# Token biases made behind the first row maxima, and two attention loads moved ahead of a larger one

## The reference

```python
def _attn_ref(q, k, v):                      # (2, 8, 768, 64) each
    k_sum = k.reshape(B, H, nb, 32, D).max(axis=3)
    v_sum = v.reshape(B, H, nb, 32, D).mean(axis=3)
    ...
    scores_all = np.concatenate([scores_l_m, scores_s], axis=-1)
    ...
    return np.matmul(a, np.concatenate([v, v_sum], axis=2))

def _moe_ref(x, modality_id, w_gate, modality_bias, w1, w2):
    logits = x @ w_gate + modality_bias[modality_id]
    e_idx = np.argmax(logits, axis=1)
    ...
            h = np.maximum(x[mask] @ w1[e], 0.0)
            out[mask] = gate_w[mask, None] * (h @ w2[e])

def _moe2_ref(x, w_in, w_out):
    h = np.maximum(x @ w_in, 0.0)
    return (h * h @ w_out).astype(np.float32)
```

## Time and profile before

| | us |
|---|---|
| three executions | 580.98, 581.5, 585.26 |
| median of them | 581.5 |
| the profiled execution, whole | 584.93 |
| its span | 583.3 |
| mean granted clock of PE in it | 0.959 |

### The profile page before, as it was taken

The page is one execution under the profiler, slowest core; times in us unless marked ns, Lnnn a source line. Parts: engine busy times, 40 slices in busy tenths (PEclk is TensorE's granted clock), DMA queues, the critical chain, the costliest instruction groups (busy, mean ns, idle before and its releaser), DMA issues.

```text
span 583.3 us, 9324 instructions
## 1 busy us (share of the span) xinstructions
PE 528.6 (91%) x3118; PEld 420.8 (72%) x3119; DVE 231.2 (40%) x434; ACT 187.5 (32%) x353; POOL 82.5 (14%) x100
## 2 busy tenths in 40 slices
PE   7878989959999699998369999999999999999996
PEld 3557778748888578786257888877888877888884
DVE  3785675966222242711552132233223224122222
ACT  1645764216221352711522222133122223122221
POOL 4423334200400040310450000011000000000000
PEclk9889988979999979999669999999999999999999
DMA  8987872691551017152220000004000001000001
GB/s 302 270 227 259 259 241 110 224 351 39 183 179 54 36 33 309 47 234 97 77 85 1 0 1 1 1 6 138 0 0 0 0 0 72 0 0 0 0 0 72
DMA packets 19272, 56.97 MB, mean 98 GB/s; under 512 B 2352, under 2 KB 2608, under 8 KB 18480
## 3 DMA queue, kind: packets, MB, share of 16 engines
q1 hardware_dynamic: 11888, 29.57, 15.9%
q0 software_dynamic: 4768, 23.60, 11.1%
q10 hardware_dynamic: 2592, 3.49, 1.6%
HBM read 42.49 MB, written 14.16 MB: 97 GB/s over the span
## 4 chain that ended last, share of the span: by engine, by line
PE 73%; issue 3%; DVE 3%; DMA 3%; ACT 3%; ACTq 1%; POOL 1%; DVEq 0%; POOLq 0%; SPq 0%
PE psum L1497 8%; PE psum L1498 8%; PE psum L1499 8%; PE psum L1478 7%; PE psum L1479 7%; PE psum L1480 7%; PE psum L1405 4%; PE psum L1406 4%; PE psum L1407 4%; PE psum L1388 4%; PE psum L1389 4%; PE psum L1390 4%; DMA x_in<-xs_d 2%; PE psum L1415 1%; ACT W L539 1%
## 5 line engine op out<-in xcount | busy, mean ns | idle before, releaser
L1187 DVE TENSOR_TENSOR sq<-r_sb 128x512 f32<-128x512 f32 x48 | 33.2, 693 | 156.7 <-ACT r_sb L650 156.7
L650 ACT ACTIVATE r_sb<-psum 128x512 f32<-128x512 f32 x48 | 28.8, 601 | 163.1 <-PE psum L1480 163.1
L1478 PE MATMUL psum<-z_hi,W 128*128 128x512 f32 x192 | 77.1, 401 | 0.8 <-DVE z_lo L1171 0.8
L1497 PE MATMUL psum<-W,s_hi 128*128 128x512 f32 x192 | 76.2, 397 | 1.1 <-DVE s_lo L1189 1.1
L1480 PE MATMUL psum<-z_hi,W 128*128 128x512 f32 x192 | 76.7, 399 | 0.0
L1479 PE MATMUL psum<-z_lo,W 128*128 128x512 f32 x192 | 76.7, 399 | 0.0
L1498 PE MATMUL psum<-W,s_hi 128*128 128x512 f32 x192 | 75.9, 396 | 0.0
L1499 PE MATMUL psum<-W,s_lo 128*128 128x512 f32 x192 | 75.8, 395 | 0.0
L1388 PE MATMUL psum<-W,x_hi 128*128 (+1 forms) x104 | 44.1, 425 | 7.6 <-DVE W L919 5.8
L1189 DVE TENSOR_TENSOR s_lo<-sq,s_hi 128x512 fp32r<-128x512 f32 x48 | 33.3, 693 | 33.6 <-ACT s_hi L652 33.6
L1405 PE MATMUL psum<-W,h_hi 128*128 (+1 forms) x104 | 42.9, 412 | 2.0 <-DVE h_lo L927 2.0
(11 more groups left out here) (198 smaller groups left out, 715.4 us busy)
## 6 DMA issues: line engine op xcount, KB each, us to landing
raw<-in_w POOLq DMA_DIRECT2D x4, 2048.0 KB, 12.3
raw<-in_w_io POOLq DMA_DIRECT2D x4, 2048.0 KB, 10.2
v_in<-in_v SPq DMA_DIRECT2D x12, 390.0 KB, 9.9
raw<-in_w SPq DMA_DIRECT2D x8, 512.0 KB, 10.2
kT<-in_kT SPq DMA_DIRECT2D x8, 400.0 KB, 7.4
q_in<-in_q SPq DMA_DIRECT2D x12, 256.0 KB, 7.9
X<-in_vT SPq DMA_DIRECT2D x2, 1536.0 KB, 14.5
x_in<-xs_d SPq DMA_DIRECT2D x12, 256.0 KB, 2.8
```

Source lines behind the costliest of these rows:

```text
L1478: pe.matmul(bank[f % 2][:, :], wh, z_hi[:, k, :], start=(k == 0), stop=False)
L1497: pe.matmul(bank[2 + j][:, :], s_hi[f % 2][:, tok], wh, start=(f == 0), stop=False)
```

## The change

In DVE's program, `bias_of_tokens()` moves from block 2 of the loop to the place behind `row_max(0)`, ahead of the loop. In SP's program, `load_v(3)` moves ahead of the second batch's vT, and `load_q(6)`, which stood behind `load_v(4)`, moves there too; in the loop that follows, the q asked for behind `load_v(i)` is that of block i + 3 instead of i + 2.

```diff
             load_q(5)
             load_v(2)
+            load_v(3)
+            load_q(6)
             load_values(1)
-            load_v(3)
             for i in range(VRING, NB):
                 load_v(i)
-                if i + 2 < NB:
-                    load_q(i + 2)
+                if i + RING < NB:
+                    load_q(i + RING)
                 if i == NBS:
                     sp.wait_ge(sem["zero"], 1)
...
             row_max(0)
+            bias_of_tokens()
             for i in range(NB):
                 if i + 1 < NB:
                     row_max(i + 1)
...
-                if i == 2:
-                    bias_of_tokens()
                 if i >= 2:
                     norm(i - 2)
```

## The result

The change makes the kernel a little faster: the median goes from 581.57 to 578.65 us (seven executions each), a ratio of 0.9935 with an interval of 0.9911 to 0.9958. The time lies in the range and within 1%, but the gain is some ten times the one forecast, and the interval of the ratio does not reach 1. The profiled execution after takes 580.0 us, the slowest of the seven; its span is 578.3, at a mean granted clock of 0.956.

The account below looks back on a forecast made before the run. PE's chain was taken to bound the kernel, with attention held up by the bias and the q_in load. A 1.3 us gain, limited by vT, and 1.0 us lost to the clock made -0.3: 581.2 us, range 578.5 to 585.2.

Parts of the forecast that it names:

- what follows attention only slides along: Stages after attention, ending near 88 us: the change touches none of them, so they only start earlier or later.
- What is late next: vT itself: Second batch's value sums: DVE waits 3.4 us for vT until 42.9, so gate(2) gains 1.3 us, not 3.87.
- the 40.5: vT's landing before the change, 23.30 + 17.2, taken from the profiled execution as the base for its new landing.
- the 2.4 us for 646 KB: DMA queue: v(3) and q(6) in front of vT delay its landing 2.4 us at 269 KB/us; bounds 0 and 2.7.
- the signs of being wrong: vT before 40.5, sum_values(1,0) without a wait, attention ending over 3 us earlier or 2 later, or changed dense stages.
- the 1.72 us for q_in: PE's wait at 44.45 for block 6's q load, expected to go because q(6) would land near 36.
- DVE's arrival: DVE reaches sum_values(1,0) at 39.45, moved by 2.15 us from 41.60, then waits for vT.
- The clock's +1.0 us: PE behind the vT wait: a hole of some 2.5 us lowers the clock and costs 1.0 us; bounds 0 and 1.7.
- The third: Rival at PE's vT wait: 1.2 GHz for twice as long costs 2.8 us; sum +1.5, 583.0 us; chance 0.18.
- the fourth: Rival: mbias late or bias still slow, row_max(1) up to 2.2 us late; 581.2 to 581.5 us; chance 0.04.
- the first (-1.3): Rival: PE's clock stays at 2.4 GHz behind the vT wait; -1.3 us, 580.2 us; chance 0.22.
- the second (-3.87): Rival: vT is not the new wait and both PE holes close; -3.87 us, 577.6 us; chance 0.08.

Follow-up runs that it names:

- the three profiles of the kernel after: The kernel with the whole change, measured three times without further edit, against the kernel before: ratios 0.9935, 0.9976 and 0.9948.
- again: The kernel before, profiled a second time with no edit: 581.24 us, span 579.6.
- all together: Kernel after with vT ahead of q(6) and v(3), sum_values(1,3) in block 5, four expert weight loads held back: 579.46 us, ratio 0.9933 against the kernel before.
- last sum: Kernel after with sum_values(1,3) moved from block 6 to block 5 on DVE: 578.78 us, ratio 0.9935 against the kernel before.
- twice: Kernel after with the six bias instructions made twice behind row_max(0): one profiled execution, 580.03 us.
- held: Kernel after with the first expert's last four weight loads held until the first token rows' scatters landed: 580.77 us, ratio 0.996 against the kernel before.

## Why the prediction was off

**Right, by the profile.** The bias costs 1.46 us at its new place (1.4 worked out), norm(0) comes at 27.20 (27.4), row_max(4) at 30.57 (30.77), mbias is there in time, and the hole in front of x_turn(0) closes. The wait for q_in goes. VT becomes what DVE waits for: 1.54, 0 and 2.76 us in the three profiles of the kernel after, where 3.4 was worked out. That what follows attention only slides along held to within the spread of single executions: from x_transpose(0) to the end it is 496.1 to 499.8 us in the fourteen profiles, before and after alike.

**The step that failed is "What is late next: vT itself"**, in its landing at 42.9. It has two terms, the 40.5 at which vT lands without the change and the 2.4 us for 646 KB put in front of it. It landed at 39.30, and two of the signs of being wrong that the forecast had named came: vT before 40.5, and an attention stage that ends over 3 us earlier. The trace records the landing of each of a transfer's 16 parts; the first, the fifteenth and the last of them for vT, in every profile:

```
moved in front of vT          first part        fifteenth         last part
nothing, v(3), v(4) next      32.10 31.84 31.33 35.85 35.05 35.97 40.52 38.00 39.09
  (before, again, bias alone)
nothing, q(6) next            31.82 31.54       35.64 34.20       35.68 35.01
  (vT first, all together)
q(6), 256 KB (v(3) behind)    33.25             37.27             37.35
v(3) and q(6), 646 KB         33.76 33.32 33.87 36.57 37.10 37.72 39.30 37.23 40.27
  (after x3, loads alone,     34.90 34.37 34.63 38.19 38.25 38.56 40.63 41.55 38.77
  last sum, twice, held)      33.93             37.95             38.65
v(3), q(6), v(4), 1036 KB     36.93             40.08             43.39
  (vT later, issued at 26.99)
```

The 2.4 us for the bytes hold for fifteen of the parts: from before's order to 646 KB in front, the mean of the first goes from 31.8 to 34.1 and that of the fifteenth from 35.6 to 37.8. What failed is the 40.5. DVE waits for the last part, and this one can stand alone behind the others: by 4.67 us in the profile of before, the widest of all, and by 2.73, 0.13 and 2.55 us in the three of the kernel after. The sum took the lag of one execution as the kernel's own; from the second profile of before, 38.00, it would have made 40.4. (The mean of the last part, 39.2 in three profiles and 39.5 in seven, does not tell 0.3 from 2.4, as single ones spread over 4 us.) The same error sits in the 1.72 us for q_in, 0.19 in the second profile of before. The forecast's own warning, that executions near 581 and near 585 exist, was applied to the total alone and not to the two landings.

The lag shows already in a load that stands in the queue ahead of those that the change moves. In the eight profiles in which the last part of vT stands 2.4 us or more behind the fifteenth, the last part of the last key load, issued near 18 us, already stands 2.1 to 3.8 us behind its own; in the other six, with at most 0.8 us at vT, it is 0.2 to 1.3. The same program has both kinds, as the three profiles of after show. So the order of the loads does not by itself decide it; what does stays open.

**DVE's arrival** was put at 39.45; it was there at 37.8 (39.33 - 1.54), because the half-speed stretch near 37 to 40 is gone too (x_turn 0.66 and values 1.15 throughout). With vT on time this earlier arrival counts, which the prediction had written off. The stretch was also longer than the two rows that the forecast counted, as a row of the kernel before shows:

```profile
36.24 1.59 PE L1228 MATMUL psum<-k_in,q_in 64*64 64x120 f32 x32
```

These scores take 1.05 us at full speed, so the stretch cost 1.5 us and not 1.0. Such a stretch lies between 30 and 40 us (granted clock 0.83) in all four profiles that lack one or both parts of the change and in three of the ten that have both; in none of the three of the kernel after.

**The clock's +1.0 us did not come.** The term was sized for a hole of 2.5 us on PE; the holes in front of gate(2) are 0.52, 0 and 0.40 us, and the matmuls behind them run at full speed. The mechanism itself is real, as the kernel with vT later still shows after a hole of 4.27 us, and also the bias alone after 3.10.

**The sum, closed.** VT 3.6 us earlier than worked out and the clock's 1.0 us not lost make 4.6 of the 4.7 us between the forecast's -0.3 and the -4.99 at gate(2), 48.02 to 43.03. Of this the span keeps 4.95. The medians show 2.9, since the profile of before stood 3.4 us above its median and that of after only 1.4: the difference between the profiles could not be carried over to the medians whole, as the forecast did.

**Rivals.** The third has a real mechanism but its hole does not arise; the fourth is refuted by the bias's 1.46 us. The result lies between the first (-1.3) and the second (-3.87). The second asked for vT by 39.45, and in two of the three profiles it was there (39.30, 37.23): what was held to need a much faster queue needs only an execution that isn't late. It is not reached in full; by the profiles some is given back: in the stop in values(3), and at x_in in front of x_transpose(0), where the wait is 2.11 and 1.41 us in the two profiles of before and 2.15, 3.30 and 4.23 in the three of after.

**Where the gain comes from.** The two waits stand in series on PE's path. Closing the first alone runs into the second (3.10 us for q_in). Closing the second alone brings no more than that wait itself, 0.19 us in the second profile of before, and leaves the first (1.99 us); what it gained by turn(6) was lost in front of x_in. The ratios of 0.9981 and 1.0008 against 0.9953 for both agree with that, though the interval of the bias alone begins at 0.9953 too, so the order of the waits is read from the profiles and not from the times. What stays open is which of the DMA's parts lags and why, and whether the instruction packet is what stops PE inside values(3).

## What to carry to other kernels

Look at a wait for a load in a second execution before its size goes into a sum: the first part of vT repeated within 0.8 us from one execution of the old order to the next, the last part did not. Where two waits stand in series and the second is for a landing, price them together, since closing the first may only lengthen the second. And follow a gain in an early stage to the next load that it meets; between the second profiles of before and after, 2.49 us in mid-attention were 0.66 at its end.

## What the runs showed of the hardware

A transfer of 1536 KB lands in 16 parts. With the DMA engines full (share 0.97 to 1.03 from 30 to 40 us), fifteen of them landed within 2.7 to 4.6 us, and the last up to 4.7 us behind these, in executions of nearly the same program, which had not been expected. With loads that dense, PE can stop in the middle of a run of 32 like matmuls for 0.30 to 1.83 us with no wait in the profile; each time it went on 1.28 to 1.55 us behind the end of a 16 KB packet of instructions. And a hole of 2.0 to 2.2 us on PE was followed by full speed in one execution (x_turn 0.63 us) and by the lower level of the clock in two (1.04 and 1.09).
